# Attention product and key moments taken head by head, and the loop over block pairs written out

## The reference, cut to what matters

```python
def phi(x):
    a = np.einsum('rd,bhsd->bhsr', S1, x)      # r = 8
    b = np.einsum('rd,bhsd->bhsr', S2, x)
    return np.einsum('bhsi,bhsj->bhsij', a, b).reshape(*x.shape[:-1], r * r)   # 64 features
q_p, k_p = (phi(q), phi(k))
kv = np.einsum('bhsf,bhsd->bhfd', k_p, v)
z = np.sum(k_p, axis=2)
num = np.einsum('bhsf,bhfd->bhsd', q_p, kv)
den = np.einsum('bhsf,bhf->bhs', q_p, z)[..., None] + 1e-06
return (num / den).astype(np.float32)
```

## Time and profile before

| what | us |
|---|---|
| median of three executions | 327.3 (326.58 to 327.33) |
| the profiled execution's own time | 327.76 |
| its span, first to last instruction | 326.0 |
| prologue, up to the first matmul of the gated layer | 42.65 |
| gated layer and attention | 42.65 to about 294 |
| mixture of experts and output | to 326.0 |

### The profile page before, as it was taken

How to read it: one execution, slowest core, us unless ns; L and a number is a source line. 1 busy time by engine, 2 the same in 40 slices (tenths; PEclk the granted TensorE clock), 3 DMA queues, 4 the chain that set the end, 5 groups by cost and what they waited for, 6 DMA issues and landing times.

```text
span 326.0 us, 6844 instructions
## 1 busy us (share of the span) xinstructions
PE 304.7 (93%) x2596; PEld 245.7 (75%) x2596; DVE 219.0 (67%) x433; ACT 176.3 (54%) x333; POOL 33.7 (10%) x51
## 2 busy tenths in 40 slices
PE   1999599999999999999999999999999999997993
PEld 0788488877888888887878888888788778895572
DVE  4576766776676758767666777676677667874374
ACT  2559255556556565654655665566546655564410
POOL 1025491010010002001000100010010001001000
PEclk9999789999999999999999999999999999999998
DMA  6996048001000000099000000000000000000008
GB/s 181 301 330 178 4 179 336 1 2 64 0 2 1 3 0 2 4 284 287 4 0 0 0 0 0 0 0 0 0 0 1 0 2 0 3 0 3 2 29 247
DMA packets 25653, 19.97 MB, mean 61 GB/s; under 512 B 4128, under 2 KB 24352, under 8 KB 25632
## 3 DMA queue, kind: packets, MB, share of 16 engines
q1 hardware_dynamic: 25632, 19.68, 20.8%
HBM read 17.45 MB, written 2.23 MB: 60 GB/s over the span
## 4 chain that ended last, share of the span: by engine, by line
PE 84%; DVE 8%; DMA 2%; ACT 2%; issue 1%; SPq 1%; POOL 0%; DVEq 0%; ACTq 0%
PE bank L858 76%; PE bank L901 2%; DVE y_nat L849 2%; DMA area<-in_k 2%; PE bank L944 1%; DVE area L665 1%; PE bank L924 1%; PE bank L881 1%; DVE hl L700 1%; PE bank L1127 1%; DVE hid L694 1%; PE bank L1021 1%; SPq L309 0%; DVE area L759 0%; SPq L311 0%
## 5 line engine op out<-in xcount | busy, mean ns | idle before, releaser
L694 DVE TENSOR_TENSOR hid<-bank,silu 128x512 f32<-128x512 f32 (+1 forms) x108 | 71.5, 662 | 71.9 <-PE bank L858 57.7
L475 ACT ACTIVATE silu<-bank 128x512 f32<-128x512 f32 (+1 forms) x108 | 61.8, 572 | 74.4 <-PE bank L858 72.8
L700 DVE TENSOR_TENSOR hl<-hid,hh 128x512 fp32r<-128x512 f32 (+1 forms) x108 | 70.7, 655 | 0.1
L483 ACT ACTIVATE hh<-hid 128x512 fp32r<-128x512 f32 (+1 forms) x108 | 64.7, 599 | 0.8 <-DVE hid L694 0.8
L858 PE MATMUL bank<-xh,wgh 128*128 128x512 f32 (+1 forms) x117 | 47.1, 403 | 0.3 <-DVE xl L843 0.3
L858 PE MATMUL bank<-xh,wgl 128*128 128x512 f32 (+1 forms) x117 | 44.4, 380 | 0.0
L858 PE MATMUL bank<-xl,wgh 128*128 128x512 f32 (+1 forms) x117 | 44.2, 378 | 0.0
L858 PE MATMUL bank<-hh,woh 128*128 128x512 f32 (+1 forms) x108 | 43.8, 405 | 0.4 <-DVE hl L700 0.4
L858 PE MATMUL bank<-hh,wol 128*128 128x512 f32 (+1 forms) x108 | 41.1, 380 | 0.0
L858 PE MATMUL bank<-xh,wvl 128*128 128x512 f32 (+1 forms) x108 | 41.1, 380 | 0.0
L858 PE MATMUL bank<-xh,wvh 128*128 128x512 f32 (+1 forms) x108 | 41.1, 380 | 0.0
(11 more groups left out here) (150 smaller groups left out, 370.4 us busy)
## 6 DMA issues: line engine op xcount, KB each, us to landing
area<-in_moe_w SPq DMA_DIRECT2D x1, 4096.0 KB, 14.3
area<-in_moe_w SPq DMA_DIRECT2D x8, 512.0 KB, 7.3
area<-in_k SPq DMA_DIRECT2D x4, 512.0 KB, 6.3
y_nat<-in_v SPq DMA_DIRECT2D x4, 512.0 KB, 6.5
q_in<-in_q SPq DMA_DIRECT2D x4, 512.0 KB, 4.3
out<-y_nat SPq DMA_DIRECT2D x8, 256.0 KB, 2.9
area<-in_moe_w_gate SPq DMA_DIRECT2D x1, 768.0 KB, 8.6
area<-in_moe_w_val SPq DMA_DIRECT2D x1, 768.0 KB, 9.3
```

The lines of the kernel that those rows point to most:

```text
L475: act.activation(silu[n][:, 0:w], gate_b[n][:, 0:w], ACT.Silu).then_inc(s_silu_ready, 1)
L483: act.activation(hh[m % NH][:, 0:w], hid[m % 2][:, 0:w], ACT.Copy).then_inc(s_hh_ready, 1)
L694: dve.tensor_tensor(hid[n][:, 0:w], val_b[n][:, 0:w], silu[n][:, 0:w], ALU.mult).then_inc(s_hid_ready, 1)
L700: dve.tensor_tensor(hl[m % NH][:, 0:w], hid[m % 2][:, 0:w], hh[m % NH][:, 0:w].bitcast(F32), ALU.subtract).then_inc(s_hl_ready, 1)
```

## The change

The zeros of `kv` go: it holds 33 columns for a pair of heads in place of 66. Each attention product is split by head, into one with rows 0 to 63 that writes `bank_a` and one with rows 64 to 127 that writes `bank_b`, with 33 moving columns each. A key moment product moves 33 columns, those of its own head. The loops on four engines are written out, `kv_now` with its copy and its wait goes, and so does the clearing of `kv` with the wait for it (`s_kvpads_ready`). VectorE reads even heads from one bank and odd heads from the other, in block 8 too, where it had one bank. The helpers that asked whether an index is a register no longer ask.

```diff
-        kv = sb("kv", [P, B, HP, 2 * DA])
-        kv_now = sb("kv_now", [P, HP, 2 * DA])
+        kv = sb("kv", [P, B, HP, DA])
...
-            pool.memset(kv[:, :, :, :], 0.0).then_inc(s_kvpads_ready, 1)
...
-            with pool.Fori(1, B) as b:
-                pool.wait_ge(s_nd_ps, b * 2)
-                pool.tensor_copy(kv_now[:, :, :], kv[:, b, :, :]).then_inc(s_kvnow_ready, 1)
+            for b in range(1, B):
...
-            with act.Fori(1, B) as b:
+            for b in range(1, B):
...
             def attention(jn):                                  # VectorE
                 nt = width(jn) // P
-                n = nt * H // 2 if nt == HT else nt * H
-                parts = ((0, bank_a), (1, bank_b)) if nt == HT else ((0, bank_a),)
+                n = nt * HP
                 dve.wait_ge(s_nd_ps, jn + 1)
-                for i, bk in parts:
+                for odd, bk in enumerate((bank_a, bank_b)):
...
-                    x_v = x_at[:, :, :].rearrange("p t (h d) -> p (t h) d", h=H)
-                    ins = dve.tensor_tensor(x_v[:, i * n:(i + 1) * n, :], nd[:, :, 0:D],
...
+                    x_v = x_at[:, 0:nt, :].rearrange("p t (hp x d) -> p (t hp) x d", hp=HP, x=2)
+                    ins = dve.tensor_tensor(x_v[:, :, odd, :], nd[:, :, 0:D],
...
-                    rows, x = slice((h % 2) * FT, (h % 2 + 1) * FT), h % 2
-                    ins = dve.tensor_copy(kv[rows, b, h // 2, x * DA:(x + 1) * DA],
-                                          mom_b[h // 2][rows, x * DA:(x + 1) * DA])
+                    rows = slice((h % 2) * FT, (h % 2 + 1) * FT)
+                    ins = dve.tensor_copy(kv[rows, b, h // 2, :], mom_b[h // 2][rows, 0:DA])
...
             def attention(jn, b):                               # TensorE
                 pe.wait_ge(s_qpT_ready, HP * jn + HP)
-                if not isinstance(b, int):
-                    pe.wait_ge(s_kvnow_ready, b)
+                whole = not (jn == NB)
                 for t in range(width(jn) // P):
                     for hp in range(HP):
-                        bk = (bank_a, bank_b)[t // 2] if whole else bank_a
-                        col = slice(((t % 2) * HP + hp) * 2 * DA, ((t % 2) * HP + hp + 1) * 2 * DA)
+                        col = slice((t * HP + hp) * DA, (t * HP + hp + 1) * DA)
                         for x, (rows, tok) in enumerate(halves(t)):
-                            moments_of = kv[:, b if whole else 2 * t + x, hp, :] if isinstance(b, int) else kv_now[:, hp, :]
-                            ins = mm(bk[rows, col], qpT[:, hp, tok], moments_of)
+                            for odd, bk in enumerate((bank_a, bank_b)):
+                                head = slice(odd * FT, (odd + 1) * FT)
+                                ins = mm(bk[rows, col], qpT[head, hp, tok], kv[head, b if whole else 2 * t + x, hp, :])
...
-                        ins = mm(mom_b[hp][x * FT:(x + 1) * FT, 0:2 * DA], kp[G % NK][:, t, h * FT:(h + 1) * FT],
-                                 v_aug[b % 2][:, G3 * g + t, 2 * hp:2 * hp + 2, :],
+                        ins = mm(mom_b[hp][x * FT:(x + 1) * FT, 0:DA], kp[G % NK][:, t, h * FT:(h + 1) * FT],
+                                 v_aug[b % 2][:, G3 * g + t, h, :],
...
-            with pe.Fori(1, B) as b:
+            for b in range(1, B):
```

More of the change, by code:

```diff
@@ L288, in later @@
         def later(count):
-            return not isinstance(count, int) or count > 0
+            return count > 0
         def later_block(j):
-            return not isinstance(j, int) or j + 2 <= NB
+            return j + 2 <= NB
         def width(j):
-            return W if not isinstance(j, int) or j < NB else P * (NT - NB * HT)
+            return W if j < NB else P * (NT - NB * HT)
         block = ctx.enter_context(nc.Block())
@@ L471, in step @@
                 jm = j if m < C else j + 1
-                if m < C or not isinstance(j, int) or j < NB:
+                if m < C or j < NB:
                     w, n, i = width(jm), m % 2, C * j + m
@@ L477, in step @@
                 jm = j if m < C else j + 1
-                if m >= 0 and (m < C or not isinstance(j, int) or j < NB):
+                if m >= 0 and (m < C or j < NB):
                     w, i = width(jm), C * j + m
@@ L645, in attention @@
                     dve.wait_ge(s_xsq_ready, jn)
-                for i, bk in parts:
+                for odd, bk in enumerate((bank_a, bank_b)):
                     nd = bk[:, 0:n * DA].rearrange("p (n d) -> p n d", d=DA)
-                    x_v = x_at[:, :, :].rearrange("p t (h d) -> p (t h) d", h=H)
-                    ins = dve.tensor_tensor(x_v[:, i * n:(i + 1) * n, :], nd[:, :, 0:D],
-                                            rden[:, i * n:(i + 1) * n].unsqueeze(2).to_broadcast([P, n, D]), ALU.mult)
-                    ins.then_inc(s_x_ready, 2 // len(parts))
+                    x_v = x_at[:, 0:nt, :].rearrange("p t (hp x d) -> p (t hp) x d", hp=HP, x=2)
+                    ins = dve.tensor_tensor(x_v[:, :, odd, :], nd[:, :, 0:D],
+                                            rden[:, odd * n:(odd + 1) * n].unsqueeze(2).to_broadcast([P, n, D]), ALU.mult)
+                    ins.then_inc(s_x_ready, 1)
             def mean_square(jn):
@@ L669, in split_x @@
                 w = width(jn)
-                if isinstance(jn, int) and jn == 0:
+                if jn == 0:
                     dve.wait_ge(s_small_loaded, 32)
@@ L720, in whole_block @@
                         logits(j - 1)
-                    if isinstance(j, int) and j == NB - 1 and c == 9:
+                    if j == NB - 1 and c == 9:
                         dve.tensor_reduce(cmax_a[:, :], logit[:, 0:NA, :].rearrange("p t s -> p s t"), axis=AX.X,
@@ L871, in queries_T @@
             def queries_T(jn, half, b):
-                if isinstance(jn, int) and jn == NB:
+                if jn == NB:
                     pe.wait_ge(s_qrem_loaded, 16 * B)
@@ L907, in attention @@
                 pe.wait_ge(s_qpT_ready, HP * jn + HP)
-                if not isinstance(b, int):
-                    pe.wait_ge(s_kvnow_ready, b)
+                whole = not (jn == NB)
                 for t in range(width(jn) // P):
                     for hp in range(HP):
-                        whole = not (isinstance(jn, int) and jn == NB)
-                        bk = (bank_a, bank_b)[t // 2] if whole else bank_a
-                        col = slice(((t % 2) * HP + hp) * 2 * DA, ((t % 2) * HP + hp + 1) * 2 * DA)
+                        col = slice((t * HP + hp) * DA, (t * HP + hp + 1) * DA)
                         for x, (rows, tok) in enumerate(halves(t)):
-                            moments_of = kv[:, b if whole else 2 * t + x, hp, :] if isinstance(b, int) else kv_now[:, hp, :]
-                            ins = mm(bk[rows, col], qpT[:, hp, tok], moments_of)
+                            for odd, bk in enumerate((bank_a, bank_b)):
+                                head = slice(odd * FT, (odd + 1) * FT)
+                                ins = mm(bk[rows, col], qpT[head, hp, tok], kv[head, b if whole else 2 * t + x, hp, :])
                 ins.then_inc(s_nd_ps, 1)
@@ L957, in gate_value @@
                     pe.wait_ge(s_xl_ready, j + 1)
-                if isinstance(i, int) and i == 1:
+                if i == 1:
                     pe.wait_ge(s_kv_ready, B)
```

7 lines of the change are left out of this document (1 added, 6 removed).

## The result

The changed kernel takes 328.56 us (median of 20 runs, 326.67 to 331.99). The kernel before, run beside it, takes 327.07 (20 runs, 326.12 to 328.00). The ratio is 1.0051, with a 95% interval of 1.0037 to 1.0066: slower by 0.5%, about 1.5 us. The slowest of the 20 runs of the changed kernel counts as a slow run and is left out of the ratio. The forecast was 327.4 us, to be counted as no difference, in a range from 324.0 to 333.0. The time lies in that range, 1.2 us above the forecast, and above the 327.0 to 327.9 that the prediction gave its likeliest case. The difference is small, and it is clear of zero.

What follows compares the result with a forecast made beforehand. TensorE, busy for 93% of the span, was taken to bound the kernel. 327.76 + 0.2 (attention) - 0.1 (key moments) = 327.9 us for the profiled execution, 0.46 above the median: 327.4 us, no difference; range 324.0 to 333.0.

Steps and rivals of the forecast that it cites:

- likeliest case: Whole kernel: no difference as summed, 327.4 us, between 327.0 and 327.9; chance 0.49.
- Part 1: Cost of one short TensorE product: streaming 66 columns 0.055 us, loading 64 stationary columns 0.057; the two level.
- Part 2: Attention product after the change: loads bind, 0.90 to 1.00 us against 0.936; +0.03 us a block, +0.2 us in all.
- columns bind: Rival, attention product and key moments: loads are hidden, halved columns give 0.40 us a block; 324.0 us, chance 0.20.
- the row groups take turns: Rival, attention product: row groups can't load at once, 0.93 us more a block; 334.9 us, chance 0.17.
- A floor between starts: Rival, attention product: 64 records can't start as close as the logits', middle 1.23 us; about 329.8 us, chance 0.10.
- Part 3: Key moments in the prologue: halved columns give nothing at 2.4 or 1.2 GHz; 0.1 us allowed over the last three groups.
- Part 4: VectorE and GpSimd: block 8's additional 0.158 and at most 0.42 us hide in 0.53 us slack; nothing comes out.
- Part 5: Written-out loops: turns cost nothing to win; some ten more instruction packets of 1.1 us each, hidden if fetched ahead; taken as 0.
- Idle time of TensorE put down to issue: Sign in the profile after: such idle time, at places differing between blocks, would be a cause not counted with.
- three rivals: Slower rivals holding 0.31: row groups taking turns (0.17), a floor between starts (0.10), written-out code coming late (330.6 us, 0.04).

Runs made afterwards that it cites:

- e10: Changed kernel with each attention product split again into 17 and 16 moving columns, doubling the weight loads; 336.51 us (one run).
- e1: Kernel before with only its four loops written out and the copy into kv_now dropped; 327.21 us, ratio 0.9992.
- e3: Changed kernel with the key moments back at 66 moving columns; 327.55 us, ratio 1.0008.
- e7: Kernel before with an unused tile of 32 bytes a partition, which moves the tiles behind it; 330.72 us, ratio 1.0103.
- e2: Changed kernel's attention by head and narrow moments, but with the loops and kv_now (33 columns) kept; 332.91 us, ratio 1.0177.
- e6: e2 with an unused tile of 32 bytes a partition, which puts the tiles behind it back; 329.79 us, ratio 1.0080.
- e4: Kernel before with only the key moments narrowed from 66 to 33 moving columns; 329.77 us, ratio 1.0075.
- e8: Changed kernel with 11 additional 512-column matmuls, results unread, ahead of the prologue's transposes of x; 327.06 us, ratio 0.9997.
- e9: Kernel before with 14 additional 512-column matmuls, results unread, ahead of the prologue's transposes of x; 325.89 us, ratio 0.9963.
- e13: e3 with one wait more, so that GpSimd subtracts only when x of block 0 is normalised; 323.41 us, ratio 0.9875.
- e11: Kernel before with one wait more, so that GpSimd subtracts only when x of block 0 is normalised; 323.03 us, ratio 0.9872.

## Why the time came within the range, and which step was wrong

**Part 1 was right in what doesn't bind.** The moving columns don't, by e10 and by the moments; that the stationary ones do rests on the loads 0.113 us apart and on the pace of the logits. For the moments: with half the moving columns a moment product went from (0.88 - 0.245) / 11 = 0.058 us to (0.84 - 0.239) / 11 = 0.055. (The prediction had 0.060 for the first, with the mean of another row, 0.224 in place of the moments' own 0.245.) The two causes stood level in the prediction, 0.057 against 0.055; the row that separated them, loads 0.113 us apart around a product of one column, was rightly given the greater weight.

**Part 2 was right.** Four tiles, two groups of rows by two of columns, work side by side: 64 records span 0.92 us from first to last start, forecast 0.90 to 1.00. The block gained 0.06 us where +0.03 was forecast; 0.02 of it are the attention. The other 0.04 are not the loops, for e1 has a block of 29.62 too. The full matmuls follow each other by 0.2287 us in the changed kernel and 0.2293 in the kernel before; over the 108 of a block that is enough for it. Why they do is open; the tiles behind `kv` lie elsewhere. The Trainium skill, TensorEngine Tiling (Array Packing), Key Properties, has different tiles load and multiply in parallel; the trace now agrees for groups of rows too.

**The rivals** "columns bind" (it needed a gap near 0.8 us) and "the row groups take turns" (2.0) both fell with the gap of 1.06. "A floor between starts" fell as it was priced, with 1.23 us or more for the 64 records; a floor of 0.015 us would fit this product and e10 alike, and only the 0.0084 of the logits, on other tiles, speaks against it. The Trainium skill, TensorE: Matmul & The Clock Gate, section "Wait — 56ns, not 53.3ns?", has starts never closer than about 25 ns; here 64 and 128 records in a row start 0.015 us apart, so the measurement decides against it for such tiles.

**Part 3 is the step that failed.** It read: "At 2.4 GHz the load of 0.057 us stays, so nothing", and for 1.2 GHz "again nothing; I allow 0.1 us". The pace is nearly as forecast: a group at 1.2 GHz takes 1.48 us, 1.53 before, and the last three gave 0.17 us where 0.1 was allowed. But pace is all that the part reckoned with. The last three groups stand ahead of the gated layer while the clock is at half, and what TensorE does in them has to do with when it rises again. With 66 columns it was up 0.2 us behind the first gate matmul in the kernel before, and ahead of it in e1, e3 and e7; with 33 it rose 2.2 to 2.7 us (e2, e6, e10), 4.0 us (changed kernel) and 5.0 us (e4) behind it, and full matmuls ran at 1.2 GHz meanwhile. The mean clocks over the whole span agree in all runs without fill or wait: 0.968 to 0.984 with 33 columns, 0.984 to 0.994 with 66. The prediction had named the stretch and its last moments, and even that full matmuls might be moved into it, but gave both the length of before. The term taken as 0 measured +2.3 us with the loops kept (e4) and about +1.4 in the changed kernel: 1.0051 against 1.0008 of e3, which differs from it in the moments alone, is 0.0043 x 327. That the moments carry the loss is shown by e3 and e4. That it all goes by way of this clock is not: of e4's 2.9 us the stretch holds some 2.4, but of the changed kernel's distance to the one before, 1.7 us by the ratios, the fill takes away only some 0.6 (e8 against e9), and that by a weak test.

**Part 4 was right.** Denominators still take 158 ns and scalings 419, with every other group of columns skipped; block 8 has two of 285 in place of one of 420, 0.15 us, hidden. The slack went from 0.53 to 0.47 us.

**Part 5 was right inside the span and missed a term outside it.** There are 22 instruction packets on q8 for 14, and nothing waited for them; blocks take no longer. But the time outside the span went from 1.76 to 2.03 us, and e1 shows the same 0.3 us for the loops alone. The prediction took what lies outside the span for fixed. Idle time of TensorE put down to issue, which it named as a sign, is there: 0.82 us at 32.69 in the changed kernel, inside its wait for x and so without cost, and 1.47 in e13. e6, which keeps the loops, has the same 0.82, so the written-out code is not its cause there.

In sum: forecast +0.1 us on the profiled execution, which came true within 0.1 (327.83), partly by luck, since its first gate matmul came 1.00 us early. That earlier start was an earlier x, from matmuls that had left the pace of 1.2 GHz by 13.17 us, where before's group at 13.56 still took 1.56 us. In the medians +1.5: some 1.4 with the narrow moments, at least 0.3 outside the span, less what the blocks win. Of the chance of 0.34 for slower, 0.31 stood on three rivals, of which none acted as priced; the one that did was not among them.

**What stays open.** That narrow moments keep the clock down longer is shown; why it does so is not. Why the loss is smaller in the changed kernel than in e4 was not settled. Nor was why the runs of it and of e8 spread over 4 to 5 us where e3's lie within 1.2; the traces show a part. How long the matmuls at the start of the program keep the pace of 1.2 GHz differs from execution to execution, and x is early or late with it. The two executions with narrow moments in which the group at 13.1 to 13.2 us was fast already (changed kernel and e6) had the transposes of x at 35.9 to 36.0 and took 327.83 and 327.62 us, in e6 the lowest of its six; in e4, at 37.67, it was 330.68, the highest of six. Whether narrow moments lengthen this first stretch as well was not tested. The reason why line 665 is held up was inferred from where it starts and ends; e11 shows that the order decides, not by what path.

## What to carry to other kernels

Before you halve the moving columns of a short full-precision product, look for two rows that tell loads from columns (loads in a row around a product of one column will do): with 64 stationary columns the halving bought 0.003 us of 0.058 a product. When you make a stage thinner on TensorE, read the granted clock of the stretch behind it too, since a thin stage can leave the full one that follows at half the clock, as it did here in all five traces; and look first for the wait in which the clock fell, which here one reordered instruction removed for 1.3%. If an edit changes the size of a tile, compare the pace of a matmul that you didn't touch before you explain the rest.

## What the hardware showed that was not expected

- **Place in memory.** With moving operands that start at a multiple of 64 bytes, 512-column matmuls follow each other by 0.233 to 0.235 us; with 32 bytes more, by 0.228 to 0.229. That is 1.0% of the whole kernel (e7), and in e2 it could have passed for a cost of the attention. The weight tiles did not move; tiles of other engines did, and which pairs of places are slow was not tried.
- **VectorE beside GpSimd.** A 128x512 multiplication of VectorE took 3.90 us when it started 0.06 us after a 128x1536 subtraction of GpSimd, and 0.69 alone. The Trainium skill, GPSIMD Engine Reference, Specifications, says that GpSimd shares its SBUF interfaces with VectorE and names instructions of VectorE with two SBUF inputs as a case of contention; this one has two, area and rstd, and the trace agrees.
- **Columns and clock.** Of two stages with the same order and nearly the same pace (1.53 and 1.48 us a group), the one with half the moving columns had the longer stretch at 1.2 GHz around it in every trace without fill or wait: 10.24 us (changed kernel, e2, e6, e10) and 13.65 (e4) against 3.41 (e7) and 6.83 (before, e1, e3).
- **Starts of short matmuls.** On four tiles records of 64 stationary columns started 0.015 us apart, 128 in a row (e10).
